# Attention and two routed expert layers on one core: how the third batch's scatters are released

## The reference

```python
attn_out = _attn_ref(**attn_kwargs)                # q, k, v: (4, 8, 576, 64), block-causal softmax, blocks of 64
B, H, S, D = attn_out.shape
x = np.ascontiguousarray(attn_out.transpose(0, 2, 1, 3)).reshape(B * S, H * D)      # 2304 x 512
x = _moe_ref(x=x, **moe_kwargs)                    # 8 experts, one per token, capacity 576
return _moe2_ref(x=x, **moe2_kwargs)               # skip gate, 8 experts, one per token, no capacity

# the core of a routed layer: the tokens of expert e, in order
h = np.maximum(xc[mask] @ w1[e], 0.0)              # 512 -> 1024
y[mask] = gate_w[mask, None] * (h @ w2[e])         # 1024 -> 512
```

## Time and profile before

| | us |
|---|---|
| median of 3 runs | 680.09 (679.43 to 680.19) |
| the profiled execution, its own time | 680.36 |
| its span, from the first to the last instruction | 678.8 |
| PE busy | 661.5 (97%) |
| DVE busy | 369.5 (54%) |
| ACT busy | 298.8 (44%) |
| POOL busy | 206.2 (30%) |
| granted TensorE clock, mean | 0.992 |

### The profile page before, as it was taken

How to read it: one execution, slowest core, us unless ns; L and a number is a source line. 1 busy time by engine, 2 the same in 40 slices (tenths; PEclk the granted TensorE clock), 3 DMA queues, 4 the chain that set the end, 5 groups by cost and what they waited for, 6 DMA issues and landing times.

```text
span 678.8 us, 17093 instructions
## 1 busy us (share of the span) xinstructions
PE 661.5 (97%) x5584; PEld 580.3 (85%) x5585; DVE 369.5 (54%) x1029; ACT 298.8 (44%) x713; POOL 206.2 (30%) x329
## 2 busy tenths in 40 slices
PE   7999999999999999999999999999999999999997
PEld 6788888788787888898899888888899899899996
DVE  3777878887888543367633367434721453411144
ACT  3777877888784122244422244113222352311233
POOL 5633436436332212322222212122122131112112
PEclk7999999999999899999999999999999999999999
DMA  8775768657532258510711148882365778711100
GB/s 169 185 193 132 199 182 216 161 128 187 130 105 76 88 126 297 189 42 24 243 63 43 47 153 305 315 316 94 121 230 176 271 282 317 261 31 48 45 18 34
DMA packets 95615, 105.89 MB, mean 156 GB/s; under 512 B 63757, under 2 KB 63757, under 8 KB 95568
## 3 DMA queue, kind: packets, MB, share of 16 engines
q1 hardware_dynamic: 84608, 81.03, 39.1%
q0 software_dynamic: 8912, 22.36, 10.2%
q10 hardware_dynamic: 2048, 1.87, 1.1%
HBM read 83.44 MB, written 28.63 MB: 165 GB/s over the span
## 4 chain that ended last, share of the span: by engine, by line
PE 92%; DMA 3%; issue 1%; DVE 1%; ACT 1%; ACTq 0%; POOL 0%; POOLq 0%; SPq 0%; DVEq 0%
PE ps L1573 33%; PE ps L1581 25%; PE ps L1468 8%; PE ps L1419 6%; PE ps L1443 5%; PE ps L1395 3%; PE ps L1475 3%; PE ps L1545 2%; PE ps L1409 2%; DMA rows<-queue 1%; PE ps L1551 1%; PE ps L1436 1%; PE ps L1559 1%; DMA queue<-pad 1%; DMA qn<-in_q 1%
## 5 line engine op out<-in xcount | busy, mean ns | idle before, releaser
L1573 PE MATMUL ps<-xT,w 128*128 128x128 f32 x1344 | 159.8, 277 | 1.2 <-issue 1.0
L1573 PEld LDWEIGHTS ps<-xT,w 128*128 128x128 f32 x1344 | 155.5, 192 | 5.1 <-issue 3.0
L1581 PE MATMUL ps<-w_hi,hT_hi 128*128 128x512 f32 x256 | 104.7, 409 | 0.5 <-DVE hT_lo L1089 0.3
L1581 PE MATMUL ps<-w_lo,hT_hi 128*128 128x512 f32 x256 | 100.3, 392 | 0.0
L1581 PE MATMUL ps<-w_hi,hT_lo 128*128 128x512 f32 x256 | 99.7, 389 | 0.0
L1300 ACT ACTIVATE hT_hi<-ps 128x512 fp32r<-128x512 f32 x64 | 37.9, 592 | 116.0 <-PE ps L1573 116.0
L1573 PE MATMUL ps<-xT,w_last 128*128 128x128 f32 x704 | 86.3, 277 | 0.3 <-issue 0.3
L1573 PEld LDWEIGHTS ps<-xT,w_last 128*128 128x128 f32 x704 | 82.3, 192 | 3.2 <-issue 2.5
L1089 DVE SCALAR_TENSOR_TENSOR hT_lo<-ps,hT_hi 128x512 fp32r<-128x512 f32 x64 | 44.2, 691 | 63.4 <-ACT hT_hi L1300 60.3
L1295 ACT ACTIVATE w_hi<-w2all 128x1024 fp32r (+1 forms) x48 | 47.0, 1046 | 62.4 <-PE ps L1581 56.5
L545 POOL DMA_INDIRECT out<-xs,idxo x32 | 37.3, 1167 | 110.2 <-DVE xs L1122 102.7
(11 more groups left out here) (198 smaller groups left out, 1028.9 us busy)
## 6 DMA issues: line engine op xcount, KB each, us to landing
w2all<-in_moe_w SPq DMA_DIRECT2D x10, 2048.0 KB, 15.2
w<-in_moe_w SPq DMA_DIRECT2D x7, 2048.0 KB, 8.9
rows<-queue POOLq DMA_DIRECT2D x36, 257.0 KB, 3.0
w2all<-in_moe_w SPq DMA_DIRECT2D x16, 512.0 KB, 4.8
w<-in_moe_w SPq DMA_DIRECT2D x12, 512.0 KB, 3.9
w_last<-in_moe_w SPq DMA_DIRECT2D x3, 2048.0 KB
qn<-in_q SPq DMA_DIRECT2D x32, 144.0 KB, 5.0
out<-pad SPq DMA_DIRECT2D x4, 1152.0 KB, 7.1
```

The lines of the kernel that those rows point to most:

```text
L1573: last = mm(hTp[j // 4][:, j % 4, :], w1s[slot][:, c, j * P:(j + 1) * P], xT[:, c, :], start=(c == 0), stop=(c == DC - 1))
L1581: last = mm(yp, h_[:, j, :].bitcast(f32r), w_[:, j, :].bitcast(f32r), start=(j + n == 0), stop=(j == FC - 1 and n == 2))
```

## The change

The wait in POOL's loop over the third batch's tiles 1 to 4 is made only before tile 2, for `pv_ready` of 4 x 14 + 3 = 59, the value that tile 2 waited for already. Tile 1's scatter goes right behind tile 0's, and those of tiles 3 and 4 right behind tile 2's.

```diff
             for i in range(1, NI):
 
-                pool.wait_ge(pv_ready, STEPS * (PAIRS - 2) + 1 + i)
+                if i == 2:
+                    pool.wait_ge(pv_ready, STEPS * (PAIRS - 2) + 3)
                 scatter_tile(B - 2, i)
```

## The result

The change takes 678.81 us (median of 20 executions, 677.24 to 681.41) against 680.44 us before (20 executions beside them, 678.46 to 683.21). The ratio is 0.9972 with a 95% interval of 0.9960 to 0.9984: faster by some 1.9 us (1.6 us from median to median), less than half of the 4.1 us forecast, and the median lies outside the range of 675.3 to 677.9. The traced execution took 677.24 us, with a span of 675.7. It is the fastest of the twenty.

The account below looks back on a forecast made before the run. TensorE bounds the kernel, idling 2.63 us at the end of attention for rows loaded after the last scatter. Saving 2.33 us idle and 1.81 clock, 4.14 in all, gives 676.2 from 680.36, median 676.0, range 675.3 to 677.9.

Parts of the forecast that it names:

- the forecast distances: POOL's third-batch scatters 1 to 4 start 1.37, 5.55, 6.83 and 8.11 us after the first one.
- moved as one block: Everything after pair 15's back products hangs on them, so all later rows come earlier by the same 4.1 us.
- the work in front of the rows stays as it is: End of attention: DVE, ACT and TensorE instructions ahead of the first queue rows keep their places; no cost booked.
- starts at 210.16 as now: POOL's third scatter of the third batch still waits for step 58's products, so its start does not move.
- TensorE is done with the products of step 62 at 219.27: End of attention: this time stays, so rows there at 218.85 wait for TensorE by 0.42 us.
- the 9% case: Last scatter lands as late as before, or any later wait eats the gain: time stays at 680.1 us, chance 9%.
- 0.73 and 0.89 us: Full-clock durations forecast on TensorE for step 63's 20 products and for the first 8 expert products.
- 1.81 are clock: Of the 4.14 us gain, 1.81 from TensorE's full clock after the rows: 0.67 + 0.54 + 0.60.
- The rival on the clock: TensorE's clock falls despite only 0.31 us of idle time: gain 2.64 us, time 677.4 us, chance 8%.
- The last scatter does not land earlier: Third batch's last three scatters hamper each other or descriptors come late; landing at 218.9, time 680.1 us, chance 9%.
- the burst overloads the software queue: Last scatter takes up to 8.3 us to land, the load comes 2.08 us later: 682.2 us, chance 5%.
- 205.98 for scatter 1: Third batch's second scatter on POOL starts near 205.98 instead of 206.79, following the first; worth nothing.

Follow-up runs that it names:

- r1: The change unchanged, traced a second time: one execution of 676.25 us.
- r16: The change, with DVE's copy of step 62's output put ahead of normalising pair 15's first rows: ratio 0.9947 to the kernel before, 676.31 us.
- r7: The change unchanged, a further trace: one execution of 678.26 us.
- r11: The change unchanged, a further trace in a later series: one execution of 678.18 us.
- r14: The kernel before, unchanged, traced a second time: one execution of 679.12 us.
- r17: The kernel before, unchanged, traced a third time: one execution of 683.53 us.
- r18: The kernel before, unchanged, traced a fourth time: one execution of 683.18 us.
- r3: The kernel before, with three plain 257 KB DMAs by SP to a scratch tensor added from scatter 2's time on: 681.17 us in one execution.
- r4: The kernel before, with two thin 1 KB scatters added on POOL right behind scatter 2: 682.97 us in one execution.

## Why the prediction was right or wrong

**The path was right.** In the traces that are not held the scatters went out at the forecast distances (1.38, 5.58, 6.85 and 8.14 us after the first in r1). The load followed 2.95 to 3.39 us after the last one's start, against 3.26 assumed, and its rows were there before TensorE was, in all nine traces. The wait for them is gone, DVE's copy is what comes next, with 0.25 us of idle time for 0.31 forecast, and r16 shows that it is the copy. Everything behind moved as one block.

**The step that failed: that the work in front of the rows stays as it is.** In the prediction's words, scatter 2 "starts at 210.16 as now" and "TensorE is done with the products of step 62 at 219.27". The forecast sent three scatters out earlier and put their cost for the work on pair 14 at nothing, without a reason; only the 9% case has room for it, with "any later wait that eats the gain", and names none. In the one traced execution of the first series this work came 1.82 us later, by TensorE's two waits for held copies of DVE (0.42 and 1.40 us). That is most of the 2.30 us by which its stretch missed the forecast; another 0.38 is in terms that were a little too small. Whether the earlier scatters bring the hold stays open: it is in one trace of the change of nine, and in none of the four of the kernel before. Without it the traced execution would have been near 675.4 us.

The later series of the change give 0.9938, 0.9946 and 0.9954, 676.4 to 676.7 us. That is a gain of 3.1 to 4.2 us, inside the forecast's range. The first series' 678.81 is about 2 us above them, which is the size of the hold. Its fastest execution of twenty took 677.24 us, where those of the later series took 674.8 to 675.7, and that fastest one is the one known to be held. That most of the first series was held would explain its timing, but only one execution was traced, so this is argued and not shown. Another cause is possible, since r7 and r11 took 678.3 and 678.2 us with nothing held, by a later start of the stretch. A first series in which the clock of before seldom fell could not by itself do it, since it is the change's own times that are high there.

**Some terms were mis-sized.** The forecast took 0.73 and 0.89 us for the 20 products and the first 8 expert products at the full clock. They take 0.80 and 1.09 in the change; the 8 had been scaled from the 24 behind them. With TensorE's wait for the copy ending 0.11 us later against the first scatter (15.52 us after it in r1, forecast 15.41), this makes the stretch 17.90 instead of 17.52 us, and the gain over the first trace of before 3.76 instead of 4.14 us. The same 8 products, and transposes that take 0.66 and not 0.44 us after idle time, make the 1.81 us booked for the clock too much: against r14's durations it is 1.38.

**A second step was wrong but does not explain the miss: "1.81 are clock" in every execution.** The forecast put it into the sum because the one trace had it. r14 had nearly the same idle time and no fall of the clock; r17 and r18 had one, r18 a longer one. By these traces the gain against an execution of the change that is not held is 2.0, 3.7, 3.8 or 4.9 us (r18 has another 0.6 behind the stretch), by what the kernel before happens to lose. The rival on the clock asked whether it might fall after the change. It never did in nine traces. The question that was left out is whether it always falls before it.

**The rivals.** "The last scatter does not land earlier" and "the burst overloads the software queue" did not come true: no landing of the last scatter in the change's nine traces was longer than about 3.3 us. The prediction's working has 205.98 for scatter 1, which is not 1.28 us behind the first but 1.37, its 1.07 and the 0.30 between two of POOL's; 1.38 was measured, and nothing hangs on it. By the rule of the Trainium skill ("SBUF — State Buffer", section "Who interferes with whom"), of a DVE instruction in its two-port mode and a GpSimd instruction the one that comes second is blocked for the whole of the other. That was the nearest to what the first trace shows, in a direction that I did not weigh: DVE waited while a scatter was under way on POOL. But the copies held read PSUM, ACT was held as well, and in eight traces with the same instructions side by side nothing was. So the runs do not support that rule as the cause.

**What stays open:** what held DVE and ACT, and why in the first series. The profile gives a source outside the core's known queues for two of the three waits. Payload alone (r3) and back-to-back scatters alone (r4) did not bring it in one trace each, which is too few for a hold that came once in nine.

## What to carry to other kernels

A DMA that is paced to be gentle can be the last link of a chain: look whether its landing, not its issue, releases the busiest engine, and where that engine's next wait would be, because that is the floor of the gain. When a part of a sum comes from a lower clock after an idle time, trace the kernel before several times first: the idle time repeats from execution to execution, the clock's fall need not. And measure between two anchors on either side of the change: here the stretch repeated within 0.03 us in eight traces, while whole executions of one kernel differed by up to 6 us.

## What the runs showed of the hardware

TensorE's clock after an idle time is not a function of its length alone. It stayed at 2.4 GHz through 2.26 us of idle time and after it (r14). In r3 it was already at 1.2 GHz at the end of 2.27 us: the granted clock of the last 0.44 us of the idle time is 0.72, which is a mix of both levels. After 2.53 us (r17), 2.63 (the first trace) and 2.79 us (r18) it was at 1.2 GHz too. In r4 it held through 3.56 us, the four transposes behind them still took 0.66 us at a clock of 0.97, and the 20 products behind those ran at 0.50. The lower clock also lasted differently long: in the first trace and in r17 it was gone by the back products, in r18 it reached into the 24 expert products. Stretches of TensorE alone, r3 first and then r4 (us, busy PE, clock, DMA share, GB/s):

```profile
221.00:221.44 0.44, 0.01 (x1) 0.72 1.02 393
```

```profile
223.35:224.00 0.65, 0.65 (x6) 0.97 0.04 13
224.00:225.30 1.30, 1.30 (x22) 0.50 0.00 0
```

Software-queue scatters of 257 KB started 1.28 us apart do not slow each other noticeably: SP's load, issued right behind the last landing, came 2.95 to 3.39 us after the start of the last of three in the nine traces of the change, and 3.00 to 3.47 us after a lone one in the four traces of before. In r4, with two thin ones in front of the last two scatters, the last took 4.21 us to land (4.30 us to the load).
